# The last twelve steps of the second network by halves of a pair, and half of the last store issued by ScalarE

## The chip, the core and the metric

The kernel runs on one core of a Trainium2 chip. Its engines are TensorE (PE in the profile, its weight loads PEld), VectorE (DVE), ScalarE (ACT), GpSimd (POOL) and SyncE (SP, which here only issues transfers). They run side by side, each through its own list of instructions, and meet at semaphores. The metric is the device time of one execution in microseconds; lower is better.

## The reference

```python
B, C, H, W = 2, 128, 384, 32
# attention: keys and values are kv, averaged over 4 x 4 windows, times w_sr
s = (q @ k.T) / sqrt(C);  a = softmax(s);  x = (a @ v).reshape(B * 12288, 128)
# first network:  128 -> 2048 -> 128
h = x @ w1_in;  g = h * cos(h);  x = g @ w1_out
# second network: 128 -> 2048 -> 128
h = x @ w2_in;  g = h * sigmoid(1.702 * h);  out = g @ w2_out
```

All of it is float32.

## The kernel before

Every product is made from three matmuls of a rounded part ("hi") and a remainder ("lo") of both operands: `product` (lines 548 to 554) issues w_lo with x_hi (L552), w_hi with x_lo (L553) and w_hi with x_hi (L554). The 24576 tokens go in 48 chunks of 512. In a network a chunk has 8 pairs of feature tiles (`PAIRS`), each tile 128 features wide, so a network is 384 steps (`STEPS`), and a pair is a tile of 128 partitions by 1024 columns (`PAIR`): two halves of 512 (`TOK`), each with its own feature tile.

A step of the second network, number j, is this chain:

- `up2(j)` on PE: two products into one of two PSUM buffers of a pair, `h2` (6 matmuls).
- `gelu(j)` on ACT (L853, L855): two activations of 128x1024 out of PSUM, first `g2_hi` (rounded), then `g2` (full), and one count on `g2_ready`.
- `lower_g2(j)` on DVE (L1027): `g2_lo` = `g2` minus `g2_hi`, 128x1024, and one count on `g2_lo_ready`. `g2_lo` lies where `g2` lies.
- `down2(j)` on PE: two products, one for each half, added into `y2_ps` (6 matmuls).

After the 8th step of a chunk, DVE transposes `y2_ps` into a block (`store_y`, L1040), and SP stores it with four transfers of 64 KB (L406). The first network's chain (`up1`, ACT and DVE for the cosine, POOL for the remainder, `down1`) has the same form.

The order is written out by hand, by slots. In slot s PE issues `up1(s)`, `down2(s - 14)`, `up2(s - 12)`, `down1(s - 3)`, as far as these numbers exist. ACT and DVE do step s - 13 of the second network in slot s. The last 30 of the 398 slots are unrolled, so a step number is a Python integer there. From slot 384 there is no `up1`, and from 387 no `down1`: the second network is alone. `FREED` is 372, the step of slot 384: after it `h2` alternates between two PSUM buffers, and `up2(j)` waits until `gelu(j - 2)` has freed its buffer.

Three more orders matter at the end. In slot 387 ACT first rounds the last chunk's input (`round_x2`, L865) and then does `gelu(374)`, and DVE makes the remainder (`split_x2`, L1033) ahead of `lower_g2(374)`. In slot 389 DVE does `lower_g2(376)` and then the transpose of chunk 46, for which `down2(376)` waits, since there is one bank `y2_ps`. SP ends with the four transfers of chunk 47 and then waits until all stores have landed (`stored`).

Of the kernel before, what the change touches and what calls it, by code (L numbers as in the profile page):

```python
# [13 lines left out]
F32 = mybir.dt.float32  # L14
# [3 lines left out]
ALU = mybir.AluOpType  # L18
ACT = mybir.ActivationFunctionType
AXIS_X = mybir.AxisListType.X  # L20

P = 128
BLK = 32
# [3 lines left out]
def steps(eng, count, unroll, head, tail):  # L27

    for i in range(head):
        yield divmod(i, unroll)
    trips = (count - head - tail) // unroll
    with eng.Fori(0, trips) as r:
        for u in range(head, head + unroll):
            yield r + u // unroll, u % unroll
    for i in range(head + trips * unroll, count):
        yield divmod(i, unroll)


def attention_and_networks(nc, q, kv, w_sr, w1_in, w1_out, w2_in, w2_out, out):
# [9 lines left out]
    TOK = 512  # L51
    SUB = TOK // P
    CHUNKS = B * N // TOK
# [4 lines left out]
    PAIR = 2 * TOK  # L58
# [8 lines left out]
    GELU = 1.702  # L67
# [26 lines left out]
    out_chunks = out.rearrange("(n m a) (j c) -> n j a m c", m=TOK // BLK, a=BLK, c=BLK)  # L94
# [16 lines left out]
    def put(name, shape, dt):  # L111
        size = 4 * math.prod(shape[1:])
        if size >= LINE:
            place[0] += -place[0] % LINE
        t = nc.alloc_sbuf_tensor_at(name, shape, dt, offset=place[0])
        place[0] += (size + 31) // 32 * 32
        assert place[0] <= base + arena_bytes, (name, place[0] - base, arena_bytes)
        return t
# [57 lines left out]
    g2, g2_lo, g2_hi, x2_hi, x2_lo = [], [], [], [], []  # L176
# [8 lines left out]
    y_blocks = [put(f"y_blocks{n}", [P, TOK], F32) for n in range(2)]  # L185
# [20 lines left out]
    def banks(first, width):  # L206
        return psum[:, first * BANK:first * BANK + width]
# [11 lines left out]
    h2 = [banks(4, PAIR), banks(0, PAIR)]  # L219
    FREED = STEPS - UP2  # L220
# [67 lines left out]
    g2_ready = sem("g2_ready")  # L288
    g2_lo_ready = sem("g2_lo_ready")
    y2_summed = sem("y2_summed")  # L290
    y_blocks_ready = sem("y_blocks_ready")
    stored = [sem(f"stored{n}") for n in range(2)]
# [9 lines left out]
    def within(r, p, lag):  # L302

        return not isinstance(r, int) or 0 <= r * BODY + p - lag < STEPS

    def buffer1(s, p):

        return s % 3 if isinstance(s, int) and s < UP2 else p % 2

    def buffer2(j):  # L310

        return (j - FREED) % 2 if isinstance(j, int) and j > FREED else 0

    with nc.Block() as block:

        @block.sync
        def _(sp):
# [83 lines left out]

            def store_y(c, n):
                sp.wait_ge(y_blocks_ready, c + 1)
                for j in range(P // BLK):
                    part = y_blocks[n][j * BLK:(j + 1) * BLK, :]
                    sp.dma_start(out_chunks[c, j],  # L406
                                 part.rearrange("a (m c) -> a m c",
                                                c=BLK)).then_inc(stored[n], 16)
# [5 lines left out]
            with sp.Fori(0, CHUNKS // 2 - 2) as r:  # L414
                for n in range(2):
                    load_next(r * 2 + (n + 2), n)
                    store_y(r * 2 + n, n)
# [131 lines left out]
        def _(pe):  # L549
            def product(dst, w_hi, w_lo, x_hi, x_lo, start, stop):  # L550

                nc.tensor.matmul(dst, w_lo, x_hi, start=start, stop=False)  # L552
                nc.tensor.matmul(dst, w_hi, x_lo, start=False, stop=False)  # L553
                return nc.tensor.matmul(dst, w_hi, x_hi, start=False, stop=stop)  # L554
# [97 lines left out]
            for b in range(B):  # L652
                final = b == B - 1
                for r, p in steps(pe, SB, ROUND, SUB + 1, 10):
                    s, static = r * ROUND + p, isinstance(r, int)
                    c, n_q, j = r * 2 + p // SUB, p // SUB, p % SUB
# [15 lines left out]
                    for h in range(2):  # L672
# [3 lines left out]
                        for t in range(KH):  # L676
                            k = (h * KH + t) * P
# [14 lines left out]
                    if not final and static and s in pieces:  # L692
                        n = pieces[s]
# [25 lines left out]
            def up2(j, p, c):  # L719

                if p % PAIRS == 0:
                    pe.wait_ge(x2_split, c + 1)
                at = buffer2(j)
                if isinstance(j, int) and j > FREED:
                    pe.wait_ge(g1_ready, 2 * STEPS)
                    pe.wait_ge(g2_ready, j - 1)
                elif isinstance(j, int) and j == 0:
                    pe.wait_ge(g1_ready, 2 * UP2)
                else:
                    pe.wait_ge(g2_ready, j)  # L730
                n = p // PAIRS % 2
                for k in range(2):
                    f = (p % PAIRS * 2 + k) * P
                    last = product(h2[at][:, k * TOK:(k + 1) * TOK], w2_in_hi[:, f:f + P],
                                   w2_in_lo[:, f:f + P], x2_hi[n][:, :], x2_lo[n][:, :],
                                   True, True)
                last.then_inc(h2_ready, 1)

            def down2(m, p, c):

                if isinstance(m, int) and m == 0:
                    pe.wait_ge(x1_ready, CHUNKS)
                elif p % PAIRS == 0:
                    pe.wait_ge(y_blocks_ready, c)
                pe.wait_ge(g2_lo_ready, m + 1)
                for k in range(2):
                    t, f = slice(k * TOK, (k + 1) * TOK), p % PAIRS * 2 + k
                    last = product(y2_ps, w2_out_hi[:, f, :], w2_out_lo[:, f, :],
                                   g2_hi[p % 2][:, t], g2_lo[p % 2][:, t],
                                   f == 0, f == FT - 1)  # L750
                if p % PAIRS == PAIRS - 1:
                    last.then_inc(y2_summed, 1)
# [12 lines left out]
        def _(act):  # L765
# [11 lines left out]
            def store_x1(c, n, n_saved):  # L777
                act.wait_ge(values_summed, c + 1)
                if n_saved is not None:
                    act.wait_ge(x1_saved[n], n_saved * 16)  # L780
                nc.scalar.activation(x_out[n][:, :], x1_ps, ACT.Copy).then_inc(x1_ready, 1)
# [34 lines left out]
            for b in range(B):  # L816
                final = b == B - 1
                for r, p in steps(act, SB, ROUND, 2 * ROUND, 10):
                    s, static = r * ROUND + p, isinstance(r, int)
                    c, j = r * 2 + p // SUB, p % SUB  # L820
# [29 lines left out]

            def gelu(j, p):
                act.wait_ge(h2_ready, j + 1)
                nc.scalar.activation(g2_hi[p % 2][:, :], h2[buffer2(j)], ACT.Silu,  # L853
                                     scale=GELU)
                nc.scalar.activation(g2[p % 2][:, :], h2[buffer2(j)], ACT.Silu,  # L855
                                     scale=GELU).then_inc(g2_ready, 1)

            def round_g1(i):
                act.wait_ge(g1_ready, i * 2 + 2)
                nc.scalar.activation(g1_hi[i % 4][:, :], g1[i % 4][:, :],  # L860
                                     ACT.Copy).then_inc(g1_hi_by_scalar, 1)

            def round_x2(c, n):
                act.wait_ge(y1_summed, c + 1)
                nc.scalar.activation(x2_hi[n][:, :], y1_ps, ACT.Copy).then_inc(x2_hi_ready, 1)  # L865
# [3 lines left out]
            for r, p in steps(act, SLOTS2, BODY, HEAD2, TAIL2):  # L869
                static = isinstance(r, int)  # L870
                if static and r * BODY + p == 3:
                    store_x1(CHUNKS - 1, (CHUNKS - 1) % 2, (CHUNKS - 1) // 2)
                c, evict = (p - DOWN1 - PAIRS) // PAIRS, p % PAIRS == DOWN1
                first = static and r * BODY + p == DOWN1 + PAIRS
                if evict and within(r, p, DOWN1 + PAIRS) and not first:
                    round_x2(r * 2 + c, c % 2)
                if within(r, p, UP2 + 1):
                    gelu(r * BODY + (p - UP2 - 1), (p - UP2 - 1) % BODY)
                filling = static and r * BODY + p < UP2
                if filling and r * BODY + p > 0:  # L880
                    count_turns(r * BODY + p, p)
                if within(r, p, 1):
                    cosine(r * BODY + (p - 1), (p - 1) % BODY)
                if within(r, p, 0) and not filling:
                    count_turns(r * BODY + p, p)
                if first:
                    round_x2(0, 0)
                if static and r * BODY + p - 2 in BY_SCALAR:
                    round_g1(r * BODY + p - 2)

        @block.vector
        def _(dve):
# [94 lines left out]
            for b in range(B):  # L987
                final = b == B - 1
                for r, p in steps(dve, SB, ROUND, 2 * ROUND if final else ROUND, 8):
                    s, static = r * ROUND + p, isinstance(r, int)  # L990
                    c, j = r * 2 + p // SUB, p % SUB
# [31 lines left out]
                                            ALU.mult).then_inc(g1_ready, 1)  # L1023

            def lower_g2(j, p):
                dve.wait_ge(g2_ready, j + 1)
                nc.vector.tensor_tensor(g2_lo[p % 2][:, :], g2[p % 2][:, :],  # L1027
                                        g2_hi[p % 2][:, :].bitcast(F32),
                                        ALU.subtract).then_inc(g2_lo_ready, 1)

            def split_x2(c, n):
                dve.wait_ge(x2_hi_ready, c + 1)
# [12 lines left out]
            for r, p in steps(dve, SLOTS2, BODY, HEAD2, TAIL2):  # L1045
                static = isinstance(r, int)
                c, evict = (p - DOWN1 - PAIRS) // PAIRS, p % PAIRS == DOWN1
# [15 lines left out]
                if (p - done) % PAIRS == 0 and within(r, p, done):  # L1063
                    c = (p - done) // PAIRS
                    store_y(r * 2 + c, c % 2,
                            None if static and r * 2 + c < 2 else r + c // 2)
                c = r * 2 + (p // PAIRS + 1)
# [23 lines left out]
```

## Time and profile before

| what | value |
|---|---|
| median of three runs | 2701.77 us (2701.04 to 2702.19) |
| the profiled execution: its time, its span | 2701.59 us, 2699.7 us |
| PE, PEld busy | 99%, 83% |
| DVE, ACT, POOL busy | 78%, 71%, 75% |
| mean granted TensorE clock | 0.999 |
| chain that ended last | PE 96%, DVE 1%, ACT 1%, POOL 1% |

The profile shows one execution. A busy share is that of the whole span. The chain that ended last is followed back from the last instruction, at each step to what released it. Times in the rows below are counted from the start of the span.

### The profile page before, as it was taken

The page shows a single profiled execution, that of the slowest core. Times are in us where ns is not written, and L with a number is a line of the kernel's source. Part 1 is how long each engine was busy: PE and PEld are TensorE (multiplying, and loading weights), DVE is VectorE, ACT ScalarE, POOL GpSimd, SP SyncE. Part 2 cuts the span into 40 slices and gives each one's busy share as a digit, 9 for nine tenths or more (in the row PEclk, how much of TensorE's full clock was granted, in tenths as well). Part 3 has the DMA queues.
Part 4 walks back from the last instruction along what each step waited for, and adds up shares of the span by engine and source line. Part 5 has one row for each costly group of instructions (what it writes and reads, how often), then busy time and mean ns, then how long its engine had stood idle before and what let it go on. Part 6 is the DMA issues. An engine that isn't in the chain of part 4 may idle for free.

```text
span 2699.7 us, 42501 instructions
## 1 busy us (share of the span) xinstructions
PE 2660.9 (99%) x13342; PEld 2254.2 (83%) x13342; DVE 2097.2 (78%) x2761; ACT 1917.9 (71%) x2473; POOL 2029.2 (75%) x1904
## 2 busy tenths in 40 slices
PE   7999999989999999999999999999999999999998
PEld 6999999977888888888888888888888888888886
DVE  6888888877777777777777777777777777777774
ACT  4777777776777777777777777777777777777775
POOL 2887677558778778787877787787778777777872
PEclk9999999999999999999999999999999999999999
DMA  7323222200000000000000000000000000000000
GB/s 193 71 48 82 71 47 48 57 20 5 16 8 16 9 14 16 8 16 8 16 8 16 8 16 12 11 16 8 16 8 16 8 16 8 16 14 10 16 4 12
DMA packets 220707, 67.64 MB, mean 25 GB/s; under 512 B 204544, under 2 KB 204672, under 8 KB 219776
## 3 DMA queue, kind: packets, MB, share of 16 engines
q1 hardware_dynamic: 220672, 67.21, 11.0%
q8 instruction: 18, 0.29, 0.0%
q14 instruction: 17, 0.14, 0.0%
HBM read 42.01 MB, written 25.17 MB: 25 GB/s over the span
## 4 chain that ended last, share of the span: by engine, by line
PE 96%; DVE 1%; ACT 1%; POOL 1%; issue 0%; SPq 0%; DMA 0%; ACTq 0%; POOLq 0%
PE psum L552 30%; PE psum L553 30%; PE psum L554 30%; PE psum L678 5%; POOL g_lo L537 0%; DVE g_lo L1027 0%; DMA kv_all<-in_kv 0%; ACT turns L843 0%; ACT g_hi L853 0%; SPq L337 0%; ACT g L855 0%; DVE g L1022 0%; ACT g_hi L860 0%; DVE neg_max L934 0%; PE psum L635 0%
## 5 line engine op out<-in xcount | busy, mean ns | idle before, releaser
L537 POOL TENSOR_TENSOR g_lo<-g,g_hi 128x512 fp32r<-128x512 f32 x768 | 1122.0, 1461 | 75.3 <-ACT g_hi L860 14.9
L1027 DVE TENSOR_TENSOR g_lo<-g,g_hi 128x1024 fp32r<-128x1024 f32 x384 | 597.8, 1557 | 437.8 <-ACT g L855 432.1
L534 POOL CAST g_hi<-g 128x512 fp32r<-128x512 f32 x754 | 534.2, 708 | 360.6 <-DVE g L1022 360.6
L853 ACT ACTIVATE g_hi<-psum 128x1024 fp32r<-128x1024 f32 x384 | 395.9, 1031 | 439.5 <-PE psum L554 439.5
L552 PE MATMUL psum<-g_hi,w_lo 128*128 128x512 f32 x1536 | 600.4, 391 | 15.5 <-POOL g_lo L537 6.3
L552 PE MATMUL psum<-x_hi,w_lo 128*128 128x512 f32 x1536 | 602.2, 392 | 1.6 <-DVE g L1022 1.5
L554 PE MATMUL psum<-x_hi,w_hi 128*128 128x512 f32 x1536 | 598.6, 390 | 0.0
L553 PE MATMUL psum<-x_lo,w_hi 128*128 128x512 f32 x1536 | 598.5, 390 | 0.0
L554 PE MATMUL psum<-g_hi,w_hi 128*128 128x512 f32 x1536 | 598.2, 389 | 0.0
L553 PE MATMUL psum<-g_lo,w_hi 128*128 128x512 f32 x1536 | 598.2, 389 | 0.0
L1022 DVE TENSOR_TENSOR g<-psum,g 128x512 f32<-128x512 f32 x768 | 490.6, 678 | 0.1
L1014 DVE SCALAR_TENSOR_TENSOR g<-turns,psum 128x1024 f32<-128x1024 int32 x384 | 463.7, 1208 | 20.2 <-ACT turns L843 20.2
L848 ACT ACTIVATE g<-g,half_pi 128x1024 f32<-128x1024 f32 x384 | 444.1, 1157 | 1.0 <-DVE g L1014 1.0
L474 POOL TENSOR_TENSOR probs<-probs,inverse 128x768 f32<-128x768 f32 x192 | 282.2, 1470 | 190.6 <-DVE inverse L979 188.5
L843 ACT ACTIVATE turns<-psum 128x1024 int32<-128x1024 f32 x384 | 396.1, 1032 | 16.6 <-PE psum L554 16.6
L855 ACT ACTIVATE g<-psum 128x1024 f32<-128x1024 f32 x384 | 394.1, 1026 | 0.0
L552 PEld LDWEIGHTS psum<-g_hi,w_lo 128*128 128x128 f32 x1536 | 288.5, 188 | 84.1 <-POOL g_lo L537 12.3
L552 PEld LDWEIGHTS psum<-x_hi,w_lo 128*128 128x128 f32 x1536 | 288.7, 188 | 71.6 <-ACT g L855 10.6
L554 PEld LDWEIGHTS psum<-x_hi,w_hi 128*128 128x128 f32 x1536 | 288.6, 188 | 60.9
L554 PEld LDWEIGHTS psum<-g_hi,w_hi 128*128 128x128 f32 x1536 | 288.6, 188 | 60.2
L553 PEld LDWEIGHTS psum<-g_lo,w_hi 128*128 128x128 f32 x1536 | 288.7, 188 | 59.2
L553 PEld LDWEIGHTS psum<-x_lo,w_hi 128*128 128x128 f32 x1536 | 288.6, 188 | 58.4
(74 smaller groups left out, 3037.3 us busy)
## 6 DMA issues: line engine op xcount, KB each, us to landing
q_blocks<-in_q SPq DMA_DIRECT2D x192, 64.0 KB, 2.2
x_dram<-x_out SPq DMA_DIRECT2D x48, 256.0 KB, 2.3
x_raw<-x_dram SPq DMA_DIRECT2D x48, 256.0 KB, 2.8
out<-y_blocks SPq DMA_DIRECT2D x192, 64.0 KB, 2.3
kv_all<-in_kv SPq DMA_DIRECT2D x4, 1536.0 KB, 11.3
kv_all<-in_kv SPq DMA_DIRECT2D x5, 1024.0 KB, 7.5
w_raw<-in_moe_w_in SPq DMA_DIRECT2D x2, 1024.0 KB, 7.1
kv_all<-in_kv SPq DMA_DIRECT2D x2, 512.0 KB, 9.6
```

Source lines behind the costliest of these rows:

```text
L534: nc.gpsimd.tensor_copy(g1_hi[p % 4][:, t], g1[p % 4][:, t]).then_inc(g1_hi_ready, 1)
L537: nc.gpsimd.tensor_tensor(g1_lo[p % 4][:, t], g1[p % 4][:, t], g1_hi[p % 4][:, t].bitcast(F32), ALU.subtract).then_inc(g1_lo_ready, 1)
L552: nc.tensor.matmul(dst, w_lo, x_hi, start=start, stop=False)
L553: nc.tensor.matmul(dst, w_hi, x_lo, start=False, stop=False)
L554: return nc.tensor.matmul(dst, w_hi, x_hi, start=False, stop=stop)
L843: nc.scalar.activation(turns[p % 4][:, :], h1[buffer1(i, p)], ACT.Copy, bias=0.25, scale=1.0 / (2 * math.pi)).then_inc(turns_ready, 1)
L848: nc.scalar.activation(g1[p % 4][:, :], g1[p % 4][:, :], ACT.Sin, bias=half_pi[:, :]).then_inc(cos_ready, 1)
L853: nc.scalar.activation(g2_hi[p % 2][:, :], h2[buffer2(j)], ACT.Silu, scale=GELU)
L855: nc.scalar.activation(g2[p % 2][:, :], h2[buffer2(j)], ACT.Silu, scale=GELU).then_inc(g2_ready, 1)
L1014: nc.vector.scalar_tensor_tensor(g1[p % 4][:, :], turns[p % 4][:, :], -2 * math.pi, h1[buffer1(i, p)], ALU.mult, ALU.add).then_inc(angle_r ...
L1022: nc.vector.tensor_tensor(g1[p % 4][:, t], h1[buffer1(i, p)][:, t], g1[p % 4][:, t], ALU.mult).then_inc(g1_ready, 1)
L1027: nc.vector.tensor_tensor(g2_lo[p % 2][:, :], g2[p % 2][:, :], g2_hi[p % 2][:, :].bitcast(F32), ALU.subtract).then_inc(g2_lo_ready, 1)
```

## The change

It does two things.

1. For steps j of 372 and above (only those of the unrolled end, so the last twelve), `gelu` issues four activations of 128x512 instead of two of 128x1024, in the order hi, full of the first half, hi, full of the second, with a count on `g2_ready` after each half; `lower_g2` issues two subtractions of 128x512, each behind its half's count; `down2` waits for each half's remainder ahead of that half's product. `until(j, k)` gives the counts, which go up by two a step from there. The wait of `up2` is counted over to the same event as before, both halves of `gelu(j - 2)`.
2. Of the four transfers of the very last chunk SP issues two, and ScalarE issues the other two, after a wait for the same transposed block. They count on the same `stored`.

```diff
+    def halves(j):
+        return isinstance(j, int) and j >= FREED
+    def until(j, k):
+        return FREED + (j - FREED) * 2 + (k + 1) if halves(j) else j + 1
...
             def store_y(c, n):
                 sp.wait_ge(y_blocks_ready, c + 1)
-                for j in range(P // BLK):
+                for j in range(P // BLK // 2 if isinstance(c, int) and c == CHUNKS - 1
+                               else P // BLK):
...
                 if isinstance(j, int) and j > FREED:
                     pe.wait_ge(g1_ready, 2 * STEPS)
-                    pe.wait_ge(g2_ready, j - 1)
+                    pe.wait_ge(g2_ready, until(j - 2, 1))
...
-                pe.wait_ge(g2_lo_ready, m + 1)
                 for k in range(2):
+                    if k == 0 or halves(m):
+                        pe.wait_ge(g2_lo_ready, until(m, k))
                     t, f = slice(k * TOK, (k + 1) * TOK), p % PAIRS * 2 + k
...
             def gelu(j, p):
                 act.wait_ge(h2_ready, j + 1)
-                nc.scalar.activation(g2_hi[p % 2][:, :], h2[buffer2(j)], ACT.Silu,
-                                     scale=GELU)
-                nc.scalar.activation(g2[p % 2][:, :], h2[buffer2(j)], ACT.Silu,
-                                     scale=GELU).then_inc(g2_ready, 1)
+                parts = (slice(0, TOK), slice(TOK, PAIR)) if halves(j) else (slice(0, PAIR),)
+                for t in parts:
+                    nc.scalar.activation(g2_hi[p % 2][:, t], h2[buffer2(j)][:, t], ACT.Silu,
+                                         scale=GELU)
+                    nc.scalar.activation(g2[p % 2][:, t], h2[buffer2(j)][:, t], ACT.Silu,
+                                         scale=GELU).then_inc(g2_ready, 1)
...
+            act.wait_ge(y_blocks_ready, CHUNKS)
+            for j in range(P // BLK // 2, P // BLK):
+                n = (CHUNKS - 1) % 2
+                part = y_blocks[n][j * BLK:(j + 1) * BLK, :]
+                nc.scalar.dma_start(out_chunks[CHUNKS - 1, j],
+                                    part.rearrange("a (m c) -> a m c",
+                                                   c=BLK)).then_inc(stored[n], 16)
...
             def lower_g2(j, p):
-                dve.wait_ge(g2_ready, j + 1)
-                nc.vector.tensor_tensor(g2_lo[p % 2][:, :], g2[p % 2][:, :],
-                                        g2_hi[p % 2][:, :].bitcast(F32),
-                                        ALU.subtract).then_inc(g2_lo_ready, 1)
+                parts = (slice(0, TOK), slice(TOK, PAIR)) if halves(j) else (slice(0, PAIR),)
+                for k, t in enumerate(parts):
+                    dve.wait_ge(g2_ready, until(j, k))
+                    nc.vector.tensor_tensor(g2_lo[p % 2][:, t], g2[p % 2][:, t],
+                                            g2_hi[p % 2][:, t].bitcast(F32),
+                                            ALU.subtract).then_inc(g2_lo_ready, 1)
```

## Rows read from the trace of the kernel before

**Rows 1.** The page's first part: busy us, share of the span, instructions of each engine.
```profile
PE 2660.9 (99%) x13342; PEld 2254.2 (83%) x13342; DVE 2097.2 (78%) x2761; ACT 1917.9 (71%) x2473; POOL 2029.2 (75%) x1904
```
**Rows 2.** Windows: stretch, us, busy us of each engine, clock, DMA share, GB/s.
```profile
2663.00:2696.00 33.00, 27.06 (x112) 19.95 (x110) 13.60 (x12) 17.96 (x19) 0.00 (x0) 1.00 0.05 8
2696.60:2698.80 2.20, 0.00 (x0) 0.00 (x0) 0.00 (x0) 0.00 (x0) 0.00 (x0) 0.93 0.70 119
```
**Rows 3.** Waits from 2663 us on: who waited for whom, total us, times, longest.
```profile
DVE g_lo L1027 <- ACT g L855: 18.1, 10, 3.0
...
PE psum L552 <- DVE g_lo L1027: 3.8, 5, 1.1
...
PE psum L552 <- DVE y_blocks L1040: 1.2, 1, 1.2
```
**Rows 4.** Timeline of PE, the end: start us, us, operation, idle before it.
```profile
2663.35 0.39 PE L554 MATMUL psum<-x_hi,w_hi 128*128 128x512 f32 x1
2664.80 0.50 PE L552 MATMUL psum<-g_hi,w_lo 128*128 128x512 f32 x1 [1.06 <-DVE g_lo L1027]
2665.14 0.39 PE L553 MATMUL psum<-g_lo,w_hi 128*128 128x512 f32 x1
...
2666.29 0.39 PE L552 MATMUL psum<-x_hi,w_lo 128*128 128x512 f32 x1
...
2667.43 0.39 PE L554 MATMUL psum<-x_hi,w_hi 128*128 128x512 f32 x1
...
2671.73 0.50 PE L552 MATMUL psum<-g_hi,w_lo 128*128 128x512 f32 x1 [1.20 <-DVE y_blocks L1040]
...
2680.67 0.39 PE L554 MATMUL psum<-x_hi,w_hi 128*128 128x512 f32 x1
...
2684.35 0.50 PE L552 MATMUL psum<-g_hi,w_lo 128*128 128x512 f32 x1 [0.53 <-DVE g_lo L1027]
...
2689.73 0.39 PE L554 MATMUL psum<-x_hi,w_hi 128*128 128x512 f32 x1
...
2694.67 0.40 PE L554 MATMUL psum<-g_hi,w_hi 128*128 128x512 f32 x1
```
**Rows 5.** Timeline of ACT: slot 387, then step 380.
```profile
2661.05 0.60 ACT L865 ACTIVATE x_hi<-psum 128x512 fp32r<-128x512 f32 x1 [3.50 <-PE psum L554]
2661.55 1.02 ACT L853 ACTIVATE g_hi<-psum 128x1024 fp32r<-128x1024 f32 x1
...
2681.10 1.03 ACT L853 ACTIVATE g_hi<-psum 128x1024 fp32r<-128x1024 f32 x1 [1.65 <-PE psum L554]
2682.02 1.02 ACT L855 ACTIVATE g<-psum 128x1024 f32<-128x1024 f32 x1
```
**Rows 6.** Timeline of DVE: slot 387, slot 389, step 380, last transpose.
```profile
2661.68 0.69 DVE L1033 TENSOR_TENSOR x_lo<-psum,x_hi 128x512 fp32r<-128x512 f32 x1 [2.87 <-ACT x_hi L865]
...
2669.83 1.23 DVE L1027 TENSOR_TENSOR g_lo<-g,g_hi 128x1024 fp32r<-128x1024 f32 x1 [2.85 <-ACT g L855]
2670.97 0.71 DVE L1040 STREAM_TRANSPOSE y_blocks<-psum 128x512 uint32<-128x512 uint32 x1
...
2683.07 1.23 DVE L1027 TENSOR_TENSOR g_lo<-g,g_hi 128x1024 fp32r<-128x1024 f32 x1 [2.36 <-ACT g L855]
...
2695.11 0.72 DVE L1040 STREAM_TRANSPOSE y_blocks<-psum 128x512 uint32<-128x512 uint32 x1 [1.75 <-PE psum L554]
```
**Rows 7.** Timeline of SP: the first, second and fourth transfer of the last store.
```profile
2695.85 0.32 SPq L406 DMA_DIRECT2D out<-y_blocks  x1
2696.21 0.49 SPq L406 DMA_DIRECT2D out<-y_blocks  x1
...
2697.30 0.49 SPq L406 DMA_DIRECT2D out<-y_blocks  x1
```
**Rows 8.** DMA issues from 2694 us on: count, size, median us to landing.
```profile
out<-y_blocks SPq DMA_DIRECT2D x4, 64.0 KB, 1.9
```
**Rows 9.** Line 406 over the whole span: issue ns, least/median/most.
```profile
L406 SPq DMA_DIRECT2D out<-y_blocks x192: 315/347/598, 682.3 to 2697.3; - x192
```

## The prediction

> **What bounds the kernel now.** I read the page's busy shares first: PE is busy 99% of the span [rows 1], so nothing off PE can matter except where PE stands still, and the change can only touch the end. Then the windows of the end: from 2663 to 2696 us PE is busy 27.06 of 33 us and POOL not at all, at a clock of 1.00 [rows 2]. The waits of that stretch say what PE stands for: five times for a remainder (3.8 us), once for the transposed block (1.2 us), while DVE itself waited ten times for ACT's second activation [rows 3]. Last I read PE's timeline. From 2664.80 to 2665.14 a matmul that restarts PE takes 0.34 us to the next start; the five unbroken ones from 2666.29 to 2667.43 take 0.228 each [rows 4]. Between the last matmul start of slot 387 (2663.35) and that of the kernel (2694.67) lie 31.32 us and 18 groups of six matmuls (ten `down2`, eight `up2`), 108 x 0.227 = 24.5 us. So 6.8 us of the end are holes and restarts; they are all that the first edit can win.
>
> The hole has one form. Step 380: last matmul of `up2` starts at 2680.67, ACT starts 0.43 later, DVE 1.97 after ACT, PE 1.28 after DVE, at 2684.35 [rows 4 to 6]: 3.68 us from PE to PE. In between PE has `down2` and `up2` of other steps, 13 x 0.227 = 2.95 us. It is a latency that is too long for a pipeline two slots deep, not a full engine: `down2(376)` to `down2(380)`, 2671.73 to 2684.35, are four slots of 3.15 us, of which PE needs 2.72 and ACT 1.94.
>
> **The halves.** Costs of a half: an ACT activation of 128x512 out of PSUM takes 0.60 us, and the next starts 0.50 after it (x_hi at 2661.05) [rows 5]; a DVE subtraction of 128x512 takes 0.69 (x_lo) [rows 6]. No row shows Silu or an SBUF-only subtraction of this size. Bounds: no less than half of a whole one (0.51 and 0.61), no more than a whole one (1.03 and 1.23). I take the rows of the same shape, 0.60/0.50 and 0.69, and the whole Silu of 1.03 fits beside the former: 0.43 us for 512 more columns.
>
> Count from A, ACT's start. The first half's full activation ends at 0.50 + 0.60 = 1.10, the second's at 1.50 + 0.60 = 2.10 (before, 1.94). DVE starts 0.03 later; its halves end at 1.82 and 2.82, and PE may start at 1.86 and 2.86 where it started at 3.25 before (0.43 less than 3.68). The four more instructions a step (two ACT, one DVE, one PE wait) cost 0.16 us on ACT and DVE each, where even a slot of 2.72 us leaves each idle; the added PE wait has `up2` queued behind it, but `down1` has such a wait ahead of each of its halves as well and its matmuls run on unbroken, so a satisfied one costs nothing.
>
> The rule that speaks against this edit: the Trainium skill, "VectorE: DVE Perf Modes", section "The TRN2 errata — SBUF-src ops pay a fixed extra latency per instruction", says that many small tiles pay a fixed cost each where a large one pays it once. By its fp32 formula, (N + 151)/0.96 ns, a half takes an estimated 691 ns. Trace and rule agree (0.69 for 512 columns, 1.23 for 1024); by both, the pair's second remainder still comes earlier, because the fixed cost is paid beside the other engine's work.
>
> Now slot by slot, on PE's clock, T being the last matmul start of `up2(j)`, A = T + 0.42.
> - `down2(374)`. ACT starts at 2661.55 behind x_hi, as before [rows 5]. Halves are ready for PE at 2663.41 and 2664.41. PE's last start is 2663.35, so the first product runs at 2663.58 with no hole; the second waits from 2664.26 to 2664.41 and restarts (+0.11). `up2(376)` starts at 2665.20, before 2666.29: 1.09 us won.
> - `down2(375)` needs its halves at 2666.57 and 2667.25; they are ready at 2665.6 and 2666.6. No wait.
> - `down2(376)` waits for the transpose of chunk 46, which DVE does behind both halves of `lower_g2(376)`. A is 2666.34 + 0.42 = 2666.76. Before, A was 2667.43 + 0.42 = 2667.85, and the transpose started 3.12 later (1.14 after the start of the remainder, 2669.83 to 2670.97) [rows 4, 6]. Now the second half starts at A + 2.13 and the transpose 0.60 behind it, at A + 2.73 = 2669.49; it ends at 2670.20, and PE starts at 2670.24 instead of 2671.73. Won so far 1.49. This hole (0.95 us) stays, because a bank and an order make it and not the size of a tile.
> - `down2(377)` to `down2(382)`. A product asks for its first half at T + 2.95 and has it at T + 0.42 + 1.86 = T + 2.28; for its second half at T + 3.63, has it at T + 3.28. Slack 0.35 us: PE runs without a break. From 2670.24, the six of `down2(376)` take 1.49, and twelve groups of 1.36 follow, to 2688.05.
> - `down2(383)` has nothing ahead of it. T = 2686.48, A = 2686.90: halves at 2688.76 and 2689.76. PE idles 0.7 us, runs three matmuls, idles 0.2, restarts; its last matmul starts at 2690.33. Before, last start 2694.67 followed T = 2689.73 by 4.94; now by 3.85.
>
> Sum of the first edit: 2694.67 - 2690.33 = 4.3 us (of the 6.8). Its bounds: 3.4 if each restart and hand-over is some 0.1 us worse than the rows say at nine places, 4.8 if halves cost what half a whole costs.
>
> **The last store.** Before, the transpose ends at 2695.83, the four issues start at 2695.85, 2696.21 (0.36 later) and, the fourth, 2697.30; a transfer lands 1.9 us after its issue [rows 6 to 8]. With two on each queue the later ones start at +0.36 instead of +1.45: by issue alone 1.09 us are won. But the DMA engines move all four transfers between 2696.6 and 2698.8 at a share of 0.70 [rows 2]: 2.2 x 0.70 = 1.54 us of work that two queues can't shorten. Packed without gaps that wins at most 0.66. No row shows a transfer issued by ACT; an issue costs SP between 0.315 and 0.598 us [rows 9], and ACT's own could cost more than either. Bounds: -0.4 (ACT's pair is late by its first use and one of the slowest issues) and +1.09. I take 0.6, nearest to the engines' bound. ACT has nothing queued behind its wait but the end of its list; SP's final wait counts the same total.
>
> The Trainium skill, "DMA: Bandwidth & Descriptors", section "Issuing engines are not separate DMA queues", says that issuing from several engines saves only the time of the sequencer. Its "Perfetto Trace Analysis", section "DMA Instruction — HWDGE (DVE, Sync)", adds that the generator of descriptors is locked by one sequencer at a time. If that lock holds between SP and ACT, this edit wins nothing (third case below).
>
> **Total.** 4.3 + 0.6 = 4.9 us of the profiled execution's 2701.59 (its span of 2699.7 and 1.89 outside it). That execution is 0.18 below the median of 2701.77; from the median the change gives 2696.8 us, 0.18% less. A measurement of this kernel tells 0.2%, 5.4 us, from no change. So the likeliest verdict is "within 0.2%", though nearly all of the evidence says that the time falls.
>
> **The rivals.**
> 1. The two queues run fully beside each other: 1.09 from the store, and the first edit at 4.3 or above. 5.4 us or more, 2696.3 us. For: 1.45 of the 3.87 us after the transpose are queued issues. Against: a DMA share of 0.70 already.
> 2. The store wins nothing or loses: the pairs take turns at making descriptors, or ACT's first transfer is slow. 4.3 + 0 to 4.3 - 0.4: 2697.5 to 2697.9. For: on SP itself an issue behind another takes 0.49, a first one 0.32 [rows 7], so something behind the queue is shared and busy.
> 3. The half remainder costs as much as the whole, 1.23. Then the second half is ready at A + 3.54 and asked for at A + 3.21: 0.44 lost at three round trips with the restart (378, 380, 382), 0.69 at each of 374, 376 and 383. 4.3 + 0.6 - 1.3 - 2.1 = 1.5 us, 2700.3. Against: x_lo's 0.69.
> 4. Slower: ACT becomes the bound. If a half activation keeps ACT as long as a whole one, 0.92 from start to start, the ten steps from 2661.55 take 40 x 0.92 = 36.8 and end at 2698.5 instead of 2692.1: +6.4, less 1.2 at the shorter last remainder and product, less 0.6 at the store, 4.6 us more: 2706.3. It decides from a spacing of 0.81 us; the row says 0.50.
>
> **Chances.** Forecast 0.60, rival 1 0.18, rival 2 0.14, rival 3 0.05, rival 4 0.03. Range 2695.6 to 2699.2: it takes in the first three with the first edit's own bounds, and leaves out rivals 3 and 4. Faster by over 0.2% (below 2696.4): rival 1 and a sixth of the forecast's cases, 0.28. Slower by over 0.2%: rival 4's dear end and an unforeseen shift in the loops, 0.03. Within: 0.69.
>
> **What would show it.** In the profile after: ACT activations of 128x512 near 0.60 us with starts 0.50 apart, remainders near 0.69, PE waits for remainders of about 1 us in all instead of 3.8, no hole between 2672 and 2688, one for the block of about 0.8 to 0.95; the last transpose near 2690.8, and the span's end 3.2 to 3.3 behind its end instead of 3.87. Wrong would be a hole in the middle of a `down2` in each slot, a remainder above 0.9 us, ACT's transfers starting well behind SP's, or PE holes that move into the loops before 2660 us.

## The result, and the profile after

The changed kernel takes 2696.98 us (median of 19 runs, 2696.14 to 2698.78) against 2701.77 us (19 runs, 2700.88 to 2703.64). The ratio is 0.9981 with a 95% interval of 0.9975 to 0.9987: faster, by 0.19%, a little less than the 0.2% named in the prediction as what one measurement can tell. The forecast was 2696.8 us.

The profiled execution took 2697.01 us, with a span of 2695.2. Against the span of before, 2699.7, that is 4.5 us, in three pieces. The last matmul of `up2(375)` starts 0.28 us later (2663.63 for 2663.35), which is scatter of the loops. From there to the kernel's last matmul PE takes 26.94 us for 31.32: 4.38 won. From the end of the last transpose to the end of the span it takes 3.49 us for 3.84: 0.35 won. (The prediction and the expectations below have 3.87 and 3.48 for these two, counted from spans rounded to 0.1 us; the trace has the spans as 2699.66 and 2695.21.)

The page's first part (busy us, share of the span, instructions) is as in [rows 1], because the end is 1% of the span:

```profile
PE 2660.4 (99%) x13342; PEld 2255.1 (84%) x13342; DVE 2097.1 (78%) x2773; ACT 1917.9 (71%) x2497; POOL 2028.6 (75%) x1904
```

The windows (stretch, us, busy us of PE, PEld, DVE, ACT, POOL, clock, DMA share, GB/s) answer to [rows 2]: PE is busy 26.61 of 28 us now, and in the last store the DMA share is 1.02 for 1.6 us, where it was 0.70 for 2.2 us.

```profile
2663.00:2691.00 28.00, 26.61 (x113) 20.46 (x111) 14.43 (x21) 19.49 (x38) 0.00 (x0) 1.00 0.06 10
2692.60:2694.20 1.60, 0.00 (x0) 0.00 (x0) 0.00 (x0) 0.00 (x0) 0.00 (x0) 1.00 1.02 164
```

The waits from 2663 us on (who for whom, total us, times, longest) answer to [rows 3]. PE waits once for a remainder and once for the block:

```profile
DVE g_lo L1049 <- ACT g L867: 12.8, 20, 2.1
...
PE psum L561 <- DVE y_blocks L1062: 0.8, 1, 0.8
PE psum L561 <- DVE g_lo L1049: 0.5, 1, 0.5
```

In PE's timeline (start us, us, operation, idle before it), which answers to [rows 4], there are four gaps and no more, from matmul start to matmul start: 2664.32 to 2664.67 (second half of step 374), 2669.32 to 2670.51 (the block), 2688.09 to 2689.02 (first half of step 383) and 2689.59 to 2690.00 (its second). The two short ones are too small for the view to print as idle; the reader finds them by the starts.

```profile
2663.63 0.39 PE L563 MATMUL psum<-x_hi,w_hi 128*128 128x512 f32 x1
...
2664.32 0.40 PE L563 MATMUL psum<-g_hi,w_hi 128*128 128x512 f32 x1
2664.67 0.50 PE L561 MATMUL psum<-g_hi,w_lo 128*128 128x512 f32 x1
...
2669.32 0.39 PE L563 MATMUL psum<-x_hi,w_hi 128*128 128x512 f32 x1
2670.51 0.50 PE L561 MATMUL psum<-g_hi,w_lo 128*128 128x512 f32 x1 [0.79 <-DVE y_blocks L1062]
...
2688.09 0.39 PE L563 MATMUL psum<-g_hi,w_hi 128*128 128x512 f32 x1
2689.02 0.50 PE L561 MATMUL psum<-g_hi,w_lo 128*128 128x512 f32 x1 [0.54 <-DVE g_lo L1049]
...
2689.59 0.40 PE L563 MATMUL psum<-g_hi,w_hi 128*128 128x512 f32 x1
2690.00 0.50 PE L561 MATMUL psum<-g_hi,w_lo 128*128 128x512 f32 x1
...
2690.57 0.40 PE L563 MATMUL psum<-g_hi,w_hi 128*128 128x512 f32 x1
```

ACT's timeline, step 383, answers to [rows 5]: the four activations take 0.59 to 0.62 us and start 0.47 to 0.49 apart.

```profile
2687.16 0.60 ACT L865 ACTIVATE g_hi<-psum 128x512 fp32r<-128x512 f32 x1 [0.65 <-PE psum L563]
2687.65 0.59 ACT L867 ACTIVATE g<-psum 128x512 f32<-128x512 f32 x1
2688.13 0.61 ACT L865 ACTIVATE g_hi<-psum 128x512 fp32r<-128x512 f32 x1
2688.60 0.62 ACT L867 ACTIVATE g<-psum 128x512 f32<-128x512 f32 x1
```

DVE's timeline, which answers to [rows 6]: a half remainder is 0.69 us, and the transpose of chunk 46 still stands behind the second half of step 376.

```profile
2669.13 0.69 DVE L1049 TENSOR_TENSOR g_lo<-g,g_hi 128x512 fp32r<-128x512 f32 x1 [0.29 <-ACT g L867]
2669.74 0.71 DVE L1062 STREAM_TRANSPOSE y_blocks<-psum 128x512 uint32<-128x512 uint32 x1
...
2688.28 0.69 DVE L1049 TENSOR_TENSOR g_lo<-g,g_hi 128x512 fp32r<-128x512 f32 x1 [1.04 <-ACT g L867]
2689.25 0.69 DVE L1049 TENSOR_TENSOR g_lo<-g,g_hi 128x512 fp32r<-128x512 f32 x1 [0.29 <-ACT g L867]
...
2691.00 0.72 DVE L1062 STREAM_TRANSPOSE y_blocks<-psum 128x512 uint32<-128x512 uint32 x1 [1.05 <-PE psum L563]
```

The issues of the last store, in the timeline of SP and ACT, answer to [rows 7]: both engines issue at the same moment, ACT's at 0.39 and 0.50 us against SP's 0.32 and 0.49.

```profile
2691.74 0.32 SPq L415 DMA_DIRECT2D out<-y_blocks  x1
2691.75 0.39 ACTq L907 DMA_DIRECT2D out<-y_blocks  x1
2692.10 0.49 SPq L415 DMA_DIRECT2D out<-y_blocks  x1
2692.18 0.50 ACTq L907 DMA_DIRECT2D out<-y_blocks  x1
```

The DMA issues (count, size, median us to landing) answer to [rows 8]: the median transfer takes longer to land than the 1.9 of before.

```profile
out<-y_blocks SPq DMA_DIRECT2D x2, 64.0 KB, 2.1
out<-y_blocks ACTq DMA_DIRECT2D x2, 64.0 KB, 2.4
```

### The profile page after: what moved, and what is told of

The parts are those of the page before. It is cut to its first block, busy times and chain, and to the rows that moved or that the text cites. A ratio compares the mean times of both kernels' runs of the same rounds, so it can differ in the third digit from the quotient of the medians.

```text
span 2695.2 us, 42537 instructions
## 1 busy us (share of the span) xinstructions
PE 2660.4 (99%) x13342; PEld 2255.1 (84%) x13342; DVE 2097.1 (78%) x2773; ACT 1917.9 (71%) x2497; POOL 2028.6 (75%) x1904
## 4 chain that ended last, share of the span: by engine, by line
PE 97%; DVE 1%; ACT 1%; POOL 1%; issue 0%; SPq 0%; DMA 0%; ACTq 0%; POOLq 0%
PE psum L561 31%; PE psum L562 30%; PE psum L563 30%; PE psum L687 5%; POOL g_lo L546 0%; DMA kv_all<-in_kv 0%; SPq L345 0%; ACT turns L853 0%; DVE neg_max L954 0%; PE psum L644 0%; DVE g L1042 0%; ACT g L858 0%; POOL probs L483 0%; ACT g_hi L872 0%; ACT g_hi L865 0%
## 5 line engine op out<-in xcount | busy, mean ns | idle before, releaser
L1049 DVE TENSOR_TENSOR g_lo<-g,g_hi 128x1024 fp32r<-128x1024 f32 (+1 forms) x396 | 598.4, 1511 | 433.0 <-ACT g L867 428.6
L865 ACT ACTIVATE g_hi<-psum 128x1024 fp32r<-128x1024 f32 (+1 forms) x396 | 397.8, 1005 | 435.7 <-PE psum L563 435.7
L867 ACT ACTIVATE g<-psum 128x1024 f32<-128x1024 f32 (+1 forms) x396 | 396.2, 1000 | 0.0
```

The lines of the kernel that those rows point to most:

```text
L865: nc.scalar.activation(g2_hi[p % 2][:, t], h2[buffer2(j)][:, t], ACT.Silu, scale=GELU)
L867: nc.scalar.activation(g2[p % 2][:, t], h2[buffer2(j)][:, t], ACT.Silu, scale=GELU).then_inc(g2_ready, 1)
L1049: nc.vector.tensor_tensor(g2_lo[p % 2][:, t], g2[p % 2][:, t], g2_hi[p % 2][:, t].bitcast(F32), ALU.subtract).then_inc(g2_lo_ready, 1)
```

## The experiments

Whole times scatter by 2 to 3 us within one kernel, so effects below 1 us are read from the traces, in two stretches: S, from the start of the last matmul of `up2(375)` to that of the kernel's last matmul, and E, from the end of the last transpose to the end of the span (taken unrounded from the trace). Where nothing in them was changed S repeats to within 0.02 us and E to within 0.01, with one exception for E, in e7, which is taken up below. All were compared with the kernel before on the same chip; e3, e5 and e7 ran once, for their traces, and have no ratio. A gap is given from matmul start to matmul start; an unbroken one is 0.23.

| kernel | S us | E us | ratio to before, 95% |
|---|---|---|---|
| before | 31.32 | 3.84 | |
| changed | 26.94 | 3.49 | 0.9981 (0.9975 to 0.9987) |
| a0_change | 26.95 | 3.48 | 0.9983 (0.9974 to 0.9992) |
| e1_halves_only | 26.96 | 3.84 | 0.9982 (0.9973 to 0.9991) |
| e2_store_only | 31.30 | 3.49 | 0.9999 (0.9990 to 1.0008) |
| e3_remainder_halves | 29.38 | 3.48 | |
| e4_transpose_between | 25.97 | 3.49 | 0.9976 (0.9967 to 0.9985) |
| e5_half_store | 26.95 | 2.70 | |
| e6_halves_earlier | 26.96 | 3.49 | 0.9980 (0.9970 to 0.9989) |
| e7_last_two_steps | 30.21 | 3.74 | |
| e8_last_step | 25.67 | 3.49 | 0.9974 (0.9965 to 0.9984) |
| e9_transpose_first | 30.79 | 3.85 | 0.9997 (0.9987 to 1.0006) |

### The changed kernel once more, and each part alone

a0_change is the changed kernel, without an edit.

> The changed kernel itself, as the yardstick for the others of this chip. Theory (latency holes of PE close, the last store is bound by the DMA engines): 4.4 us from the last up2(375) matmul to the last matmul of the kernel, 0.4 us behind the last transpose, in all 4.5 to 5 us below the kernel before. Rival (the gain is in part a chance shift of the loops, where the one profile stood 0.28 us later): the span up to slot 387 differs from before by more than 1 us.

S and E came out the same to 0.01 us, and `up2(375)` ended at 2663.03 instead of 2663.35: the loops are untouched, and the 0.28 us of the first profile were scatter. The rival falls.

e1_halves_only takes the second part of the change back:

```diff
-                for j in range(P // BLK // 2 if isinstance(c, int) and c == CHUNKS - 1
-                               else P // BLK):
+                for j in range(P // BLK):
...
-            act.wait_ge(y_blocks_ready, CHUNKS)
-            for j in range(P // BLK // 2, P // BLK):
...
```

> The halves stay, SP issues all four transfers of the last store. Theory: last up2(375) matmul to last matmul 26.9 us as in the changed kernel, from the end of the last transpose to the end of the span 3.87 us again, so 4.4 us below before. Rival (the two parts lean on each other, as when ACT's second queue disturbs the end): the stretch of PE differs from 26.9 by over 0.2 us, or the end is not 3.87.

S is 26.96, and E is 3.84 as before, with SP's four issues as long as before (timeline of SP):

```profile
2691.78 1.94 SPq L414 DMA_DIRECT2D out<-y_blocks  x4
```

e2_store_only takes the first part back:

```diff
     def halves(j):
-        return isinstance(j, int) and j >= FREED
+        return False
```

> No halves, ACT issues two of the last four transfers. Theory: PE's stretch is 31.3 us as before, the end 3.48 us instead of 3.87, in all 0.4 us below before, too little to tell by the times alone. Rival (a descriptor lock that the changed kernel's timing happened to miss): issues of ACT start over 0.3 us behind SP's and the end stays at 3.87.

S is 31.30 and E 3.49, the issues of both engines start at the same 2695.55 us, and the time can't be told from before. So the parts add: 4.36 to 4.38 us from the halves, 0.35 from the store. The rival's signs, ACT's issues over 0.3 us behind SP's and no gain in E, are both absent.

### Which half-sized work matters

e3_remainder_halves: ACT does whole pairs, the rest goes by halves.

```diff
-                    pe.wait_ge(g2_ready, until(j - 2, 1))
+                    pe.wait_ge(g2_ready, j - 1)
...
             def gelu(j, p):
...
-                for t in parts:
...
+                nc.scalar.activation(g2_hi[p % 2][:, :], h2[buffer2(j)], ACT.Silu,
+                                     scale=GELU)
+                nc.scalar.activation(g2[p % 2][:, :], h2[buffer2(j)], ACT.Silu,
+                                     scale=GELU).then_inc(g2_ready, 1)
...
-                    dve.wait_ge(g2_ready, until(j, k))
+                    dve.wait_ge(g2_ready, j + 1)
```

> ACT does whole pairs again (two activations of 128x1024, one count), only the remainders and the products go by halves. From ACT's start the halves of the remainder end at 2.66 and 3.26, PE can start them at 2.70 and 3.30 and asks for them at 2.53 and 3.21. Theory (one chain of latencies, each part of it counts by what it adds to the half asked for): PE's stretch from up2(375) to its end is 28.3 to 29.0 us, between the 26.9 of the changed kernel and the 31.3 of before, with small holes of 0.1 to 0.3 us at steps 378, 380, 382 and 0.5 us more than the changed kernel at 374 and at 383. Rival A (the activations' halves bring all, since DVE was idle): 31 us. Rival B (the remainders' halves bring all): 27 us.

S is 29.38, above the expected 28.3 to 29.0, and far from either rival: 1.94 us come from the remainders' halves alone and 2.43 more from those of the activations. The miss is the block's gap, which the expectation had left out: 1.66, 0.47 above the changed kernel's 1.19 and even above the 1.58 of before, since the transpose stands behind both half remainders, and two of them in a row take 0.06 us more than the whole one (1.29 for 1.23). The rest is as expected: the gap at 374 is 0.92, 0.57 above the changed kernel's, those at 378, 380 and 382 are 0.43, 0.41 and 0.38 (0.15 to 0.20 above an unbroken 0.23), and from the last `up2` matmul (2689.67) to the end (2694.06) it takes 4.39 us, 0.55 above it. In PE's timeline:

```profile
2665.60 0.50 PE L561 MATMUL psum<-g_hi,w_lo 128*128 128x512 f32 x1 [0.53 <-DVE g_lo L1047]
...
2672.63 0.50 PE L561 MATMUL psum<-g_hi,w_lo 128*128 128x512 f32 x1 [1.27 <-DVE y_blocks L1060]
...
2692.81 0.50 PE L561 MATMUL psum<-g_hi,w_lo 128*128 128x512 f32 x1 [1.10 <-DVE g_lo L1047]
```

e7_last_two_steps starts the halves at step 382, e6_halves_earlier at 356 (the first unrolled one); both have `HALVED` in place of `FREED` in `halves` and `until`, and

```diff
                 else:
-                    pe.wait_ge(g2_ready, j)
+                    pe.wait_ge(g2_ready, until(j - 1, 1))
```

> Halves only for the last two steps, 382 and 383. Theory (each hole is closed by the halves of its own step alone): the holes at 374, 376, 378 and 380 stay as before (1.45, 1.58, 0.96, 0.92 us from start to start), that at 382 is gone and the last shrinks, so the stretch is 29.3 to 29.5 us: 1.9 of the 4.4 us come from the last two steps. Rival (a hole that is closed reopens one step later, the pipeline only shifts): the stretch is within 0.5 us of 31.3 less the 1.1 of the last step.

My theory fell, its rival stands: S is 30.21, 1.1 us won and not 1.9. The gap ahead of `down2(382)` is gone (PE's timeline, 2689.51 to 2689.74), but that of step 383 is only what it is with all halves, 0.93 and then 0.40:

```profile
2689.51 0.39 PE L564 MATMUL psum<-x_hi,w_hi 128*128 128x512 f32 x1
2689.74 0.39 PE L562 MATMUL psum<-g_hi,w_lo 128*128 128x512 f32 x1
...
2690.87 0.39 PE L564 MATMUL psum<-g_hi,w_hi 128*128 128x512 f32 x1
2691.80 0.50 PE L562 MATMUL psum<-g_hi,w_lo 128*128 128x512 f32 x1 [0.54 <-DVE g_lo L1050]
```

While PE stood at `down2(382)` before, the chain of step 383 (started by `up2(383)`, ahead of it in PE's order) was running already. The hole of 382 was part of the time that 383 had to wait anyway, so the two are one: 4.94 us from the last `up2` matmul to the end [rows 4], 3.84 now. Closed holes may be added only where a new `up2` starts between them.

> The halves begin at step 356 instead of 372, so for 16 more steps, in which the first network still runs and PE has 4.08 or 5.4 us of work a slot. Theory (there PE has no hole to close, and ACT and DVE have idle time for the fixed costs): the same time as the changed kernel within 0.5 us, PE's start of step 375's last matmul in place within 0.5 us, PE's stretch behind it 26.9. Rival (fixed costs of 0.16 us a step on ACT and DVE, DVE beside a busy POOL, delay the first network's chain, as its remainders of 128x512 took up to 1.09 us there): PE gets holes before 2660 us and the time rises by 1 us or more.

S is 26.96, `up2(375)` ends at 2662.81 (2663.03 to 2663.65 in the others of clock 1.00 with the same halves), and PE waits for nobody between 2580 and that point. In these 16 steps, where PE has enough to do, half-sized work gives and costs nothing that shows.

### The store

e5_half_store: SP and ACT issue one transfer each; two quarters of the last chunk's output are left out.

```diff
-                for j in range(P // BLK // 2 if isinstance(c, int) and c == CHUNKS - 1
+                for j in range(1 if isinstance(c, int) and c == CHUNKS - 1
...
-            for j in range(P // BLK // 2, P // BLK):
+            for j in range(P // BLK // 2, P // BLK // 2 + 1):
...
-                sp.wait_ge(stored[n], LOADS * (CHUNKS // 2))
+                sp.wait_ge(stored[n], LOADS * (CHUNKS // 2) - n * LOADS // 2)
```

> The changed kernel without two of the last four transfers: SP and ACT issue one each, at the same moment, and half of the last chunk isn't stored. Theory (after the first issues the DMA engines' work sets the end, some 0.38 to 0.41 us for each 64 KB transfer): the end behind the last transpose is 2.6 to 2.8 us instead of 3.48. Rival (issue by issue: the end is the last issue's start plus its landing): the last issue starts 0.43 us earlier, so the end is 3.05.

E is 2.70: two transfers fewer are worth 0.79 us, 0.39 each. That is close to their time on the DMA engines (1.6 us at a share of 1.02 for four in the changed kernel, so 0.41 each) and nearly twice the 0.43 us by which the last issue starts earlier. So after the change the engines' work bounds the store. A transfer with one other beside it lands after 1.9 (SP) and 2.2 us (ACT); with three beside it the first of each engine lands after 2.0 and 2.3, the second after 2.3 and 2.6.

```profile
out<-y_blocks SPq DMA_DIRECT2D x1, 64.0 KB, 1.9
out<-y_blocks ACTq DMA_DIRECT2D x1, 64.0 KB, 2.2
```

In e7, whose edit has no part in the store, E is 3.74, where the seven other profiles with all four transfers and two issuers have 3.48 or 3.49. Its trace says where the 0.25 us arose: ACT's second issue starts 0.72 us after its first and not 0.43, and E grows by nearly all of these 0.29. So the last issue has hardly any slack against the engines' work. Why ACT was late there stays open.

```profile
2694.53 0.39 ACTq L908 DMA_DIRECT2D out<-y_blocks  x1
2695.25 0.32 ACTq L908 DMA_DIRECT2D out<-y_blocks  x1
```

### What is left, and two better versions

e4_transpose_between moves the transpose of chunk 46 between the halves of the remainder of step 376:

```diff
                 for k, t in enumerate(parts):
+                    if k == 1 and j == STEPS - PAIRS:
+                        store_y(CHUNKS - 2, 0, (CHUNKS - 2) // 2)
                     dve.wait_ge(g2_ready, until(j, k))
...
-                if (p - done) % PAIRS == 0 and within(r, p, done):
+                if (p - done) % PAIRS == 0 and within(r, p, done) and not (
+                        static and r * BODY + p == done + (CHUNKS - 2) * PAIRS):
```

> The changed kernel, with the transpose of chunk 46 moved in DVE's order from behind lower_g2(376) to between its two halves. Theory (what is left of the hole at slot 390 is DVE's order and not the chain of latencies): the hole of 1.19 us between PE starts ahead of down2(376) (0.96 more than a running matmul) closes to 0.0 to 0.2, and the time falls by another 0.9 to 1.1 us, to 5.7 us below before. Rival (PE waits there for the chain of activations anyway): the second half of the remainder is 0.4 us late and half or more of the hole comes back in the middle of down2(376) or at the next steps, so that less than 0.5 us is won.

The hole is gone: PE goes from 2670.80 to 2671.02 unbroken, but for a restart of 0.31 right behind it. S falls by 0.98 us to 25.97, as the theory had it, and nothing comes back in the middle of `down2(376)` or later. DVE's timeline shows the order:

```profile
2669.62 0.69 DVE L1051 TENSOR_TENSOR g_lo<-g,g_hi 128x512 fp32r<-128x512 f32 x1 [1.31 <-ACT g L867]
2670.23 0.71 DVE L1064 STREAM_TRANSPOSE y_blocks<-psum 128x512 uint32<-128x512 uint32 x1
2670.86 0.65 DVE L1051 TENSOR_TENSOR g_lo<-g,g_hi 128x512 fp32r<-128x512 f32 x1
```

e9_transpose_first puts the same transpose ahead of the whole `lower_g2(376)` in the kernel before (`store_y` called at the head of `lower_g2`, and no longer behind it).

> The kernel before, whole pairs and one issuer of the store, with the transpose of chunk 46 ahead of lower_g2(376) on DVE. Theory (the hole at slot 390 has two walls, DVE's order and behind it the step's own latency): the hole from start to start falls from 1.58 to 0.95-1.0 us, and the time by 0.6 us, against 0.98 us in the changed kernel, because there the halves had taken the second wall down. Rival (the order alone makes the hole): it closes and 1.3 us are won without any halves.

The gap falls from 1.58 to 1.05 us and S by 0.53, each a little short of what was expected (0.95 to 1.0, and 0.6), and the wait has another name (PE's timeline):

```profile
2669.49 0.39 PE L554 MATMUL psum<-x_hi,w_hi 128*128 128x512 f32 x1
2670.54 0.47 PE L552 MATMUL psum<-g_hi,w_lo 128*128 128x512 f32 x1 [0.67 <-DVE g_lo L1029]
```

So the hole had two walls. Moving one without halves is worth 0.53, moving it with them 0.98.

e8_last_step adds to e4 another order in step 383: ACT makes the full activations of both halves first, DVE rounds the first half itself.

```diff
+                if isinstance(j, int) and j == STEPS - 1:
...
+                    nc.scalar.activation(g2[p % 2][:, t0], x[:, t0], ACT.Silu,
+                                         scale=GELU).then_inc(g2_ready, 1)
+                    nc.scalar.activation(g2[p % 2][:, t1], x[:, t1], ACT.Silu, scale=GELU)
+                    nc.scalar.activation(g2_hi[p % 2][:, t1], x[:, t1], ACT.Silu,
+                                         scale=GELU).then_inc(g2_ready, 1)
+                    return
...
+                    if k == 0 and isinstance(j, int) and j == STEPS - 1:
+                        nc.vector.tensor_copy(g2_hi[p % 2][:, t],
+                                              g2[p % 2][:, t]).then_inc(last_hi, 1)
+                        dve.wait_ge(last_hi, 1)
```

> The kernel with the transpose moved between the halves, and in step 383 another order: ACT makes the full activation of both halves first and then the rounded one of the second; DVE rounds the first half itself, ahead of its remainder. Counted from ACT's start the first product may then start at 1.78 us instead of 1.86 and the second is ready at 2.38, before it is asked for (2.58). Theory (what is left at the last step is only its own chain ACT, DVE, PE): one hole of 0.85 us from start to start, none in the middle, the last matmul 0.3 to 0.4 us earlier after the last up2 matmul (3.84 now), the stretch 25.6 instead of 25.97. Rival (DVE's rounding is as long as a remainder, 0.69, with the hand-over to itself): the first product starts at 2.1 and the end wins under 0.1 us.

S is 25.67 (25.6 expected), another 0.30 less, with one gap of 0.91 (0.85 expected) and none in the middle. DVE's rounding takes 0.43 us:

```profile
2686.54 0.43 DVE L1061 CAST g_hi<-g 128x512 fp32r<-128x512 f32 x1 [0.56 <-ACT g L866]
2687.00 1.29 DVE L1064 TENSOR_TENSOR g_lo<-g,g_hi 128x512 fp32r<-128x512 f32 x2
```

This is the best version that was tried: 2695.34 us (10 runs) against 2702.55 of the kernel before on the same chip, ratio 0.9974. By the traces it is 6.0 us below before (5.65 in S, 0.35 in E), 1.3 of them beyond the change. Its interval overlaps that of the changed kernel, so the whole times alone don't rank the two; the stretches do.

One order was left untested. In every `down2` PE waits for the remainder ahead of three matmuls, of which the first and the third (`g_hi,w_lo` and `g_hi,w_hi`) read only the rounded half. In the changed kernel ACT has made that of step 383 at 2687.76 (2687.16 and 0.60), and PE starts at 2689.02. With the wait behind these two, part of what is left at step 383 might go as well.

## Why the prediction was right

- **The end is a latency too long for the pipeline.** Right. S was forecast as 26.98 us (2690.33 less 2663.35), and is 26.94.
- **Costs of a half.** 0.60/0.50 and 0.69 were taken from a copy and a subtraction out of PSUM; Silu takes 0.59 to 0.62 with 0.47 to 0.49 between starts, the remainder 0.69. The price of halving a pair was put at 0.16 us on ACT and on DVE; it is 0.12 on ACT (2.06 us from the first start to the last end, for 1.94) and 0.15 on DVE (2 x 0.69 for 1.23), only 0.06 where DVE does both halves in a row (e3), and it is paid beside PE's work. The fixed cost that the Trainium skill warns of (the section cited in the prediction) is there, then, and does no harm here.
- **Step 374.** 1.09 us forecast; the gap fell from 1.45 to 0.35, so 1.10.
- **The block's hole.** PE was to start again 6.89 us after `up2(375)`'s last matmul; it does after 6.88. That the hole is made by DVE's order was argued only. e4 shows it, and e9 shows that it holds only once the halves are there.
- **Steps 377 to 382.** Unbroken, as forecast; e3 shows that the slack of 0.35 us needs both edits: without the activations' halves each round trip has a gap of 0.38 to 0.43, start to start.
- **Step 383.** Gaps of 0.93 and 0.41, forecast as 0.7 and 0.2 of idling, each above the 0.23 of a running matmul. My working by the clock had this right; the reading behind rival 3 and behind e7, that each hole has a price of its own which can be added, was wrong, as e7 shows.
- **The last store: the size was off.** 0.6 forecast, 0.35 measured; the span's end comes 3.49 us behind the transpose's, forecast as 3.2 to 3.3. The bound by the DMA engines was the right one (e5), but the working counted only their stretch of work. That shrank from 2.11 us (in the trace, first packet to last; the 2.2 of [rows 2] has edges with nothing in them) to 1.60, so by 0.51 and not 0.66, and the work itself rose from 1.54 to 1.6 x 1.02 = 1.63. The time from the last packet to the span's end, which the working took as unchanged, grew from 0.86 to 1.02. Seen from the issues: the last one starts 1.01 us earlier (0.46 after the transpose's end for 1.47), and 0.66 of this went back, as a second transfer lands 2.3 (SP) and 2.6 us (ACT) after its issue, where the last of before took 1.9.
- **The lock** (rival 2, a rule of the Trainium skill, "Perfetto Trace Analysis", section "DMA Instruction — HWDGE (DVE, Sync)") doesn't show as one that is held for a whole issue. That the two issues start together says little, since a wait could lie inside them; their lengths say more: SP's are those of SP alone (0.32 and 0.49), ACT's are 0.39 and 0.50, so at most 0.07 us of waiting fits in. Something does hold ACT's transfers back, though: issued at the same moment as SP's, the first one moves its first data 0.2 us later (in the changed kernel only SP's queue has packets up to 2692.78, from 2692.58 on) and lands 0.3 later. No run has ACT issue alone, so whether this is sharing or ACT's own price stays open. The rule of the Trainium skill, "DMA: Bandwidth & Descriptors", section "Issuing engines are not separate DMA queues", that several issuers save only issue time, is borne out as an upper bound: 1.0 us of issue time saved, 0.35 us of it kept.
- **Total.** 4.9 forecast; 4.5 by the spans, 4.7 by the two stretches (4.38 and 0.35), 4.8 by the medians. That the medians come within 0.2 us of the forecast is in part luck, with runs of one kernel up to 2.8 us apart. "Within 0.2%" was the likeliest verdict, and 0.19% is what came.

## What to carry to other kernels

Where an engine waits on a chain of others and none of them is full, count the chain from the last matmul to the first that needs it, and compare it with the work in between; cutting the tiles pays by what the *first asked-for* piece gains, and only until the chain fits. Don't add up closed holes: two holes with one chain running beneath them are one hole. When an engine's list has an instruction that somebody waits for behind one that waits itself, put it into the wait.

## What the runs showed of the hardware

- In the first 60 us lies a difference between profiles that has nothing to do with the change. In those of e4 and e3 the granted TensorE clock is at its lower level, 1.2 GHz (0.50 of the full 2.4), for 3.4 us, from 38.1 (e3: 37.6) to 41.5 us (41.0), and at the full level on both sides; in that of a0_change, as in the nine others, it stays at the full level there. Ahead of the fall PE was busy 1.29 of 3.3 us in e4, 1.71 in e3, but 2.13 in a0_change. Half of 3.4 us is 1.7, an estimate of what this costs while PE is busy. `up2(375)` ends at 2665.09 us in e4, at 2664.68 in e3 and between 2662.7 and 2663.7 in the ten others, 2663.2 in the mean: 1.9 and 1.5 later. Windows of e4 and then of a0_change (columns as above; the clock is the third from the right):

```profile
34.70:38.00 3.30, 1.29 (x6) 0.98 (x6) 2.99 (x8) 1.61 (x5) 1.37 (x1) 1.00 1.04 218
38.10:41.40 3.30, 3.25 (x12) 2.96 (x13) 1.89 (x5) 1.86 (x4) 1.87 (x1) 0.50 1.13 185
```

```profile
34.70:38.00 3.30, 2.13 (x13) 1.82 (x14) 2.69 (x8) 1.77 (x4) 2.36 (x2) 1.00 1.06 227
38.10:41.40 3.30, 2.92 (x18) 2.28 (x16) 2.86 (x7) 2.90 (x7) 2.37 (x2) 1.00 1.03 200
```

  The whole times fit this: of 33 runs of the kernel before beside a0_change, 20 lie between 2700.69 and 2702.34 and 13 between 2703.08 and 2703.86, with medians 1.5 us apart. That this stretch makes the two groups is argued and not shown, and what sets the clock there stays open.
- ACT's first transfer of the kernel takes 0.39 us to issue, less than its second (0.50) and 0.07 more than SP's first; it lands after 2.3 us, SP's after 2.0. In e7, where ACT's second starts 0.33 us after the end of its first, it takes 0.32.
- Two queues bring the 16 DMA engines from a share of 0.70 to 1.02 with 64 KB transfers in pieces of 128 bytes; 164 GB/s is what they moved then, 119 before.
